# A gated linear attention whose decays come from a forward and a backward scan, feeding two MLPs: a change to how the decays are made and to the order of the opening

## The chip, the cores and the metric

The kernel runs on one core of a Trainium2 chip. The metric is the device time of one execution in microseconds (us). The engines are TensorE (PE in the profile, with PEld for its weight loads), VectorE (DVE), ScalarE (ACT), GpSimd (POOL) and SyncE (SP, which here only issues transfers). ACT issues transfers too; a transfer that an engine issues is marked with a q behind the engine's name (ACTq, SPq).

## The reference

```python
# q, k, v, f_logit: (4, 8, 768, 48), float32
f = 1 / (1 + exp(-f_logit))
for t in range(768):
    state = f[:, :, t, :, None] * state + k[:, :, t, :, None] * v[:, :, t, None, :]
    y[:, :, t] = einsum('bhd,bhde->bhe', q[:, :, t], state)
x = y as (3072 tokens, 384)
x = ((sigmoid(x @ w_gate)) * (x @ w_val)) @ w_out          # d_ff 1536
h = x @ w_in;  out = (h * sigmoid(1.702 * h)) @ w_out2     # d_ff 2048
```

## The kernel before, in words

The attention is cut into 48 units. A unit is one pair of heads (2 x 48 rows of state, laid on partitions 0 to 47 and 64 to 111) and 256 tokens, which are four chunks of C = 64 tokens. UG = 4 pairs make the 384 rows of x for 256 tokens, so units 0 to 3 make the first 256 tokens of x, units 4 to 7 the next.

For a unit, ACT takes the sigmoid of the gates (`forget`), DVE scans them into a running product that starts anew at each chunk (`begin_decay`, L804) and takes the reciprocal of all 256 products (`end_decay`, L811). POOL multiplies q by the products (`decay_q`, L506) and k by their reciprocals (`decay_k`, L514). `prepare(n)` on DVE is both steps, `decay(n)` on POOL both multiplications. `take_end` on ACT keeps each chunk's whole product in p_end; `prepare_q` multiplies q by the end of the chunk before.

TensorE does the attention in 50 visits. Visit v can do three things for three units (`VISITS[v]`): turn k of unit n and make its scores (it needs k_dec, then q_dec), make the chunks' key-value products of unit n-1, and make the outputs of unit n-2 (it needs the masked scores and the states, which DVE makes in `mask` and `new_states` after a visit, in `after_visit`). After some visits of the opening TensorE multiplies an identity on nothing (`keep_warm`: 8 times after visits 6 and 7). Visits 0 to 7 come ahead of the MLPs: visits 0 to 3 turn units 0 to 3, visit 4 makes the products of unit 3, visits 5 and 6 the outputs of units 2 and 3, and visit 7 turns unit 4.

Outputs y go by DMA into x_raw. The MLPs run behind it, block by block: a block is 128 hidden rows for one group of tokens (the first two groups have 256 tokens, the others 512). Every fp32 operand is split into a high part (ACT) and the rest (DVE, or POOL for the first weight piece and for w2), and each product is three matmuls (L1087 to L1089). TensorE's order in a block of the first MLP is: gate, value, a visit if one is due, and the output product of the block before. The sequences of all engines are written out by hand, one after another in each engine's function, so an instruction that waits holds back all that stands behind it on its engine. `PREPARE_AT`, `FORGET_AT` and `VISIT_AT` say in which blocks `prepare`, `forget` and the later visits stand. The gates' first two and the other loads of the opening stand in ACT's and SP's sequences.

The weights of the first MLP come in 12 pieces. Piece t is loaded by ACT (`load_w1`), cast (`w1_first_part`) and finished by DVE (`w1_second_part`), piece 0 in thirds by POOL (`split_w1`), and block 0 waits for these.

Of the kernel before, what the change touches and what calls it, by code (L numbers as in the profile page):

```python
# [12 lines left out]
P = 128  # L13
# [3 lines left out]
def gla_moe_moe2(nc, q_t, k_t, f_t, v_n, v_t, w1, w2, out_t, x_dram, x2_dram):  # L17
# [68 lines left out]
    with ExitStack() as ctx:  # L86
# [33 lines left out]
        gate = sb("gate", [P, 2, W])  # L120
        floor = sb("floor", [P, 2, W])
        prod = sb("prod", [P, 2, W])
        inv_prod = sb("inv_prod", [P, 2, W])
# [32 lines left out]
        gate_done = sem("gate_done")  # L156
        scan_done = sem("scan_done")
        inv_done = sem("inv_done")
# [148 lines left out]
        def end_before(u, c):  # L307

            return p_end[:, u.n, c - 1:c] if c else p_end[:, u.n - UG, CH - 1:CH]
# [57 lines left out]
        with nc.Block() as block:  # L367

            @block.sync
            def _(sp):  # L370
# [7 lines left out]
                def load_kq(n):  # L378
                    if n < UNITS:
                        u = Unit(n)  # L380
                        wait(sp, q_dec_done, n - 1)
                        for i in range(PAIR):
                            sp.dma_start(q_raw[rows[i], u.s, :], q_t[u.pair, i, :, u.tokens]).then_inc(q_loaded[u.s], 16)
                        wait(sp, k_dec_done, n - 1)
                        for i in range(PAIR):
                            sp.dma_start(k_raw[rows[i], u.s, :], k_t[u.pair, i, :, u.tokens]).then_inc(k_loaded[u.s], 16)
# [48 lines left out]
                move_y(3, slice(1, None))  # L435
                load_f(7)
# [49 lines left out]
            def _(pool):  # L486
# [8 lines left out]
                                   pattern=[[1, C]], channel_multiplier=-1).then_inc(steps_set, 1)  # L495
                pool.wait_ge(steps_set, 3)
# [3 lines left out]
                def decay_q(n):  # L500
# [5 lines left out]
                    pool.tensor_tensor(q_dec[:, n % 4, :], q_raw[:, u.s, :], prod[:, u.s, :], ALU.mult).then_inc(q_dec_done, 1)  # L506

                def decay_k(n):
                    u = Unit(n)
                    pool.wait_ge(k_loaded[u.s], (u.uses + 1) * 32)  # L510
                    pool.wait_ge(inv_done, n + 1)
                    if n >= 2:
                        pool.wait_ge(visit_done, turn_visit[n - 2] + 1)
                    pool.tensor_tensor(k_dec[:, u.s, :], k_raw[:, u.s, :], inv_prod[:, u.s, :], ALU.mult).then_inc(k_dec_done, 1)  # L514

                def decay(n):
                    if n < UNITS:
                        decay_q(n)
                        decay_k(n)
# [38 lines left out]
            def _(act):  # L558
# [19 lines left out]
                def forget(n):  # L578
# [7 lines left out]
                    f_c = f_raw[:, u.s, :].rearrange("p (c t) -> p c t", c=CH)  # L586

                    act.activation(gate[:, u.s, :].rearrange("p (c t) -> p c t", c=CH)[:, :, 1:C], f_c[:, :, 1:C], ACT.Sigmoid)
                    act.activation(floor[:, u.s, :].rearrange("p (c t) -> p c t", c=CH)[:, :, 0], f_c[:, :, 0],
                                   ACT.Sigmoid).then_inc(gate_done, 1)  # L590
# [18 lines left out]
                def take_end(n):  # L609

                    act.wait_ge(scan_done, n + 1)
                    act.copy(p_end[:, n, :],
                             prod[:, n % 2, :].rearrange("p (c t) -> p c t", c=CH)[:, :, C - 1]).then_inc(p_end_done, 1)

                def prepare_q(n):
# [44 lines left out]
                act.activation(y_t[:, 0, 0:1], x_raw[:, 0, 0:1], ACT.Sigmoid)  # L660
                first_load_f(1)
# [26 lines left out]
                first_load_f(6)  # L688
                load_w1(2)
# [4 lines left out]
                first_move_y(3, slice(0, 1))  # L694
                w1_first_part(1)
# [91 lines left out]
            def _(dve):  # L787

                dve.memset(f_raw[:, :, :], 30.0).then_inc(gaps_set, 1)
                dve.memset(q_raw[:, :, :], 0.0).then_inc(gaps_set, 1)  # L790
                dve.memset(k_raw[:, :, :], 0.0).then_inc(gaps_set, 1)
                dve.memset(gate[:, :, :], 0.0).then_inc(gaps_set, 1)
                dve.memset(floor[:, :, :], SAFE_PRODUCT).then_inc(gaps_set, 1)
                dve.memset(no_state[:, :], 0.0).then_inc(gaps_set, 1)
# [4 lines left out]
                def begin_decay(n):  # L799
                    u = Unit(n)  # L800
                    dve.wait_ge(gate_done, n + 1)
                    wait(dve, q_dec_done, n - 1)
                    wait(dve, p_end_done, n - 1)
                    dve.tensor_tensor_scan(prod[:, u.s, :], gate[:, u.s, :], floor[:, u.s, :], 1.0, ALU.mult,  # L804
                                           ALU.max).then_inc(scan_done, 1)

                def end_decay(n):
                    u = Unit(n)
                    dve.wait_ge(scan_done, n + 1)
                    wait(dve, k_dec_done, n - 1)  # L810
# [399 lines left out]
```

## Time and profile before

| | |
|---|---|
| median of 3 runs | 950.77 us (950.76 to 953.5) |
| the profiled execution | 953.08 us, of which the span of instructions is 951.0 us |
| TensorE busy | 934.9 us of the span |
| VectorE busy | 487.0 us |
| ScalarE busy | 375.3 us |
| GpSimd busy | 105.8 us |
| mean granted clock of TensorE | 0.996 |

Times below are microseconds from the start of the span unless marked otherwise. Busy time is time in which an engine has an instruction at work; the idle time in brackets stands before an instruction, with what ended it.

### The profile page before, as it was taken

How to read it: one execution, taken by the hardware profiler on the slowest of the kernel's cores; microseconds unless marked ns; L12 is line 12 of the kernel's file. 1: busy time of each engine (PE TensorE's matmuls, PEld its weight loads, DVE VectorE, ACT ScalarE, POOL GpSimd, SP SyncE). 2: the span in 40 equal slices, each digit the busy share in tenths (PEclk: the TensorE clock that was granted, in tenths of full speed). 3: DMA queues.
4: the chain of work that ended last, by engine and by line, in shares of the span. 5: the costliest groups of instructions: out<-in, count | busy, mean ns of one | idle time of the engine just before them, and what ended most of it. 6: DMA issues, size and time to landing. Idle time of an engine off the chain costs nothing.

```text
span 951.0 us, 18139 instructions
## 1 busy us (share of the span) xinstructions
PE 934.9 (98%) x7203; PEld 781.2 (82%) x7203; DVE 487.0 (51%) x829; ACT 375.3 (39%) x941; POOL 105.8 (11%) x125
## 2 busy tenths in 40 slices
PE   7899999999999999999999999999999999999997
PEld 5899988888888888888888888888888888888885
DVE  7897776647665665664333234343443443433433
ACT  4665444543444444443424333233232333232332
POOL 4211211101110111110004420000000000000000
PEclk9899999999999999999999999999999999999999
DMA  5762322211112212120123320020010200100000
GB/s 146 201 188 60 85 64 61 64 47 58 57 48 54 80 52 51 29 80 21 63 69 98 99 84 1 1 67 1 24 43 1 68 1 1 66 1 1 34 1 35
DMA packets 44008, 52.36 MB, mean 55 GB/s; under 512 B 8464, under 2 KB 33808, under 8 KB 43920
## 3 DMA queue, kind: packets, MB, share of 16 engines
q1 hardware_dynamic: 41184, 43.30, 15.8%
q10 hardware_dynamic: 2736, 7.85, 2.9%
q8 instruction: 59, 0.97, 0.4%
q14 instruction: 29, 0.24, 0.1%
HBM read 36.96 MB, written 9.44 MB: 49 GB/s over the span
## 4 chain that ended last, share of the span: by engine, by line
PE 95%; DVE 2%; issue 1%; ACT 1%; DMA 1%; SPq 0%; ACTq 0%; POOL 0%; DVEq 0%; POOLq 0%
PE up_ps L1087 17%; PE up_ps L1088 17%; PE up_ps L1089 17%; PE out_ps L1087 13%; PE out_ps L1088 12%; PE out_ps L1089 12%; PE att_ps L1035 2%; PE att_ps L1057 1%; PE att_ps L1047 1%; PE turn_ps L1014 1%; PE up_ps L1003 1%; PE att_ps L1069 1%; PE att_ps L1080 1%; DMA x_raw<-y_t 1%; DVE inv_prod L811 1%
## 5 line engine op out<-in xcount | busy, mean ns | idle before, releaser
L1087 PE MATMUL up_ps<-x_hi,w_hi 128*128 128x512 f32 (+1 forms) x792 | 293.7, 371 | 1.5 <-DVE x_lo L867 0.8
L1089 PE MATMUL up_ps<-x_hi,w_lo 128*128 128x512 f32 (+1 forms) x792 | 293.2, 370 | 0.0
L1088 PE MATMUL up_ps<-x_lo,w_hi 128*128 128x512 f32 (+1 forms) x792 | 293.1, 370 | 0.0
L1087 PE MATMUL out_ps<-act_hi,w_hi 128*128 128x512 f32 (+1 forms) x540 | 208.0, 385 | 0.8 <-DVE act_lo L932 0.8
L1088 PE MATMUL out_ps<-act_lo,w_hi 128*128 128x512 f32 (+1 forms) x540 | 203.2, 376 | 0.0
L1089 PE MATMUL out_ps<-act_hi,w_lo 128*128 128x512 f32 (+1 forms) x540 | 202.9, 376 | 0.0
L718 ACT CAST act_hi<-act_f 128x512 fp32r<-128x512 f32 (+1 forms) x180 | 106.6, 592 | 232.1 <-DVE act_f L923 159.7
L932 DVE TENSOR_TENSOR act_lo<-act_f,act_hi 128x512 fp32r<-128x512 f32 (+1 forms) x180 | 118.1, 656 | 113.8 <-ACT act_hi L718 113.8
L1087 PEld LDWEIGHTS up_ps<-x_hi,w_hi 128*128 128x128 f32 x792 | 149.7, 189 | 27.8 <-DVE x_lo L867 1.3
L1089 PEld LDWEIGHTS up_ps<-x_hi,w_lo 128*128 128x128 f32 x792 | 149.6, 189 | 25.3
L1088 PEld LDWEIGHTS up_ps<-x_lo,w_hi 128*128 128x128 f32 x792 | 149.7, 189 | 25.0
L926 DVE TENSOR_TENSOR act_f<-act_f,up_ps 128x512 f32<-128x512 f32 x96 | 66.0, 688 | 173.3 <-ACT act_f L714 173.3
L714 ACT ACTIVATE act_f<-up_ps 128x512 f32<-128x512 f32 x96 | 57.4, 598 | 192.9 <-PE up_ps L1089 192.9
L1087 PEld LDWEIGHTS out_ps<-act_hi,w_hi 128*128 128x128 f32 x540 | 101.8, 188 | 22.2 <-DVE act_lo L932 1.2
L1089 PEld LDWEIGHTS out_ps<-act_hi,w_lo 128*128 128x128 f32 x540 | 102.0, 189 | 18.6
L1088 PEld LDWEIGHTS out_ps<-act_lo,w_hi 128*128 128x128 f32 x540 | 102.0, 189 | 16.9
L923 DVE TENSOR_TENSOR act_f<-act_f,up_ps 128x512 f32<-128x512 f32 (+1 forms) x84 | 50.3, 599 | 112.5 <-PE up_ps L1089 103.9
L811 DVE RECIPROCAL inv_prod<-prod 128x256 f32<-128x256 f32 x48 | 84.1, 1752 | 1.6
L712 ACT ACTIVATE act_f<-up_ps 128x512 f32<-128x512 f32 (+1 forms) x84 | 45.1, 537 | 62.7 <-PE up_ps L1089 60.7
L506 POOL TENSOR_TENSOR q_dec<-q_raw,prod 128x256 f32<-128x256 f32 x48 | 35.3, 735 | 299.6 <-DVE prod L804 229.9
L639 ACT COPY y_t<-att_ps 48x128 f32<-48x128 f32 x128 | 33.3, 260 | 60.3 <-DVE state L840 59.2
L624 ACT ACTIVATE q_in<-q_dec,p_end 128x64 f32<-128x64 f32 x176 | 47.4, 339 | 0.9
(77 smaller groups left out, 577.7 us busy)
## 6 DMA issues: line engine op xcount, KB each, us to landing
stage<-w SPq DMA_DIRECT2D x16, 384.0 KB, 3.3
stage<-w ACTq DMA_DIRECT2D x9, 576.0 KB, 4.3
q_raw<-q_t SPq DMA_DIRECT2D x96, 48.0 KB, 1.9
k_raw<-k_t SPq DMA_DIRECT2D x96, 48.0 KB, 1.9
v_raw<-v_n SPq DMA_DIRECT2D x48, 96.0 KB, 2.2
x_raw<-x_dram SPq DMA_DIRECT2D x6, 768.0 KB, 5.0
out_t<-final SPq DMA_DIRECT2D x18, 256.0 KB, 2.1
f_raw<-f_t SPq DMA_DIRECT2D x82, 48.0 KB, 1.9
```

The costliest lines, as they stand in the source:

```text
L506: pool.tensor_tensor(q_dec[:, n % 4, :], q_raw[:, u.s, :], prod[:, u.s, :], ALU.mult).then_inc(q_dec_done, 1)
L624: last = act.mul(q_in[:, n % 2, at], q_dec[:, n % 4, at], end_before(u, c))
L712: act.activation(act_f[:, b.t, 0:b.n], up_ps[:, 0, 0:b.n], ACT.Sigmoid).then_inc(sig_done, 1)
L714: act.activation(act_f[:, b.t, 0:b.n], up_ps[:, b.j % 2, 0:b.n], ACT.Sigmoid, scale=1.702).then_inc(sig_done, 1)
L718: act.copy(act_hi[:, b.t, 0:b.n], act_f[:, b.t, 0:b.n]).then_inc(act_hi_done, 1)
L811: dve.reciprocal(inv_prod[:, u.s, :], prod[:, u.s, :]).then_inc(inv_done, 1)
L923: dve.tensor_tensor(act_f[:, b.t, 0:b.n], act_f[:, b.t, 0:b.n], up_ps[:, 1, 0:b.n], ALU.mult).then_inc(mul_done, 1)
L926: dve.tensor_tensor(act_f[:, b.t, 0:b.n], act_f[:, b.t, 0:b.n], up_ps[:, b.j % 2, 0:b.n], ALU.mult).then_inc(mul_done, 1)
L932: dve.tensor_tensor(act_lo[:, b.t, 0:b.n], act_f[:, b.t, 0:b.n], act_hi[:, b.t, 0:b.n].bitcast(F32), ALU.subtract).then_inc(act_split, 1)
L1087: pe.matmul(dst, w_hi[:, at:at + P], m_hi, start=first, stop=False)
L1088: pe.matmul(dst, w_hi[:, at:at + P], m_lo, start=False, stop=False)
L1089: return pe.matmul(dst, w_lo[:, at:at + P], m_hi, start=False, stop=last)
```

## The change

The product up to a token and its reciprocal are replaced by two scans. One runs backwards over the chunk and gives, for each token, the product of the gates behind it (`after_prod`), which k takes. The other runs forwards, but starts each chunk at one over the chunk's whole product, and q takes it (`to_prod`). Four reciprocals per unit, one for each chunk, are left of the 256. The buffers get two columns per chunk for the starts and ends (264 instead of 256 elements). The sigmoid is one instruction instead of two. On POOL, k comes before q. The states and q_in are decayed by the chunk's own product (`end_of`) instead of the one before. `begin_decay` is now the backward scan with the four reciprocals, `end_decay` the forward scan; in the MLP's blocks the first stands ahead of `after_visit`, the second behind it. The opening's sequences on SP, POOL, ACT and DVE are written anew.

```diff
@@ POOL
+pool.memset(starts[:, :, :], SAFE_PRODUCT).then_inc(starts_set, 1)
+pool.memset(no_state[:, :], 0.0).then_inc(starts_set, 1)
+pool.memset(starts[...][:, :, :, C + 1], 1.0).then_inc(starts_set, 1)
 def decay_q(n):
-    pool.tensor_tensor(q_dec[:, n % 4, :], q_raw[:, u.s, :], prod[:, u.s, :], ALU.mult)
+    pool.tensor_tensor(by_chunk(q_dec[:, n % 4, :]), by_chunk(q_raw[:, u.s, :]), chunks(to_prod, u.s)[:, :, 1:C + 1],
+                       ALU.mult)
 def decay_k(n):
-    pool.wait_ge(inv_done, n + 1)
-    pool.tensor_tensor(k_dec[:, u.s, :], k_raw[:, u.s, :], inv_prod[:, u.s, :], ALU.mult)
+    pool.wait_ge(after_done, n + 1)
+    pool.tensor_tensor(by_chunk(k_dec[:, u.s, :]), by_chunk(k_raw[:, u.s, :]), chunks(after_prod, u.s)[:, :, 2:],
+                       ALU.mult)
 def decay(n):
-        decay_q(n)
         decay_k(n)
+        decay_q(n)
 decay(3)
-pool.wait_ge(state_done, CH * 2)
 split_w1(0)
 split_w1(1)
+decay_k(4)
+split_w1(2)
 decay_q(4)
-pool.wait_ge(state_done, CH * 4)
-split_w1(2)
-decay_k(4)
 decay(5)
@@ ACT
-    act.activation(gate...[:, :, 1:C], f_c[:, :, 1:C], ACT.Sigmoid)
-    act.activation(floor...[:, :, 0], f_c[:, :, 0], ACT.Sigmoid).then_inc(gate_done, 1)
+    act.activation(chunks(gate, u.s)[:, :, 1:C + 1], by_chunk(f_raw[:, u.s, :]), ACT.Sigmoid).then_inc(gate_done, 1)
+act.wait_ge(gaps_set, 2)
 first_load_f(1)
 forget(0)
 first_load_f(2)
 forget(1)
-first_load_f(3)
 take_end(0)
 take_k(0)
+first_load_f(3)
 forget(2)
-first_load_f(4)
 take_end(1)
+take_k(1)
 prepare_q(0)
-take_k(1)
 forget(3)
 load_w1(0)
-prepare_q(1)
 take_end(2)
 take_k(2)
-first_load_f(5)
+prepare_q(1)
+take_end(3)
 w1_first_part(0)
+take_k(3)
 take_y(0)
-take_end(3)
-take_k(3)
+prepare_q(2)
 load_w1(1)
-prepare_q(2)
 forget(4)
 take_y(1)
 prepare_q(3)
-first_load_f(6)
-load_w1(2)
 forget(5)
 take_y(2)
 first_move_y(2, slice(2, None))
 take_y(3)
 first_move_y(3, slice(0, 1))
+load_w1(2)
 w1_first_part(1)
@@ SP: k before q in load_kq; load_f(4), load_f(5), load_f(6) added ahead of load_kq(4), load_kq(5) and load_f(7)
@@ DVE
-dve.memset(f_raw[:, :, :], 30.0)
+dve.memset(f_raw[:, 0, :], 30.0)
+dve.memset(f_raw[:, 1, :], 30.0)
-dve.memset(floor[:, :, :], SAFE_PRODUCT)
-dve.memset(no_state[:, :], 0.0)
 def begin_decay(n):
-    wait(dve, q_dec_done, n - 1)
-    dve.tensor_tensor_scan(prod[:, u.s, :], gate[:, u.s, :], floor[:, u.s, :], 1.0, ALU.mult, ALU.max)
+    wait(dve, k_dec_done, n - 1)
+    dve.tensor_tensor_scan(after_prod[:, u.s, ::-1], gate[:, u.s, ::-1], starts[:, u.s, ::-1], 1.0, ALU.mult, ALU.max)
+    dve.wait_ge(after_done, n + 1)
+    dve.reciprocal(chunks(starts, u.s)[:, :, 0], chunks(after_prod, u.s)[:, :, 1]).then_inc(start_done, 1)
 def end_decay(n):
-    wait(dve, k_dec_done, n - 1)
-    dve.reciprocal(inv_prod[:, u.s, :], prod[:, u.s, :]).then_inc(inv_done, 1)
+    wait(dve, q_dec_done, n - 1)
+    dve.tensor_tensor_scan(to_prod[:, u.s, :], gate[:, u.s, :], starts[:, u.s, :], 1.0, ALU.mult, ALU.max)
 prepare(0)
 prepare(1)
+begin_decay(2)
 after_visit(0)
-prepare(2)
+end_decay(2)
+begin_decay(3)
 after_visit(1)
-prepare(3)
+end_decay(3)
 after_visit(2)
-begin_decay(4)
 after_visit(3)
 after_visit(4)
-end_decay(4)
-begin_decay(5)
 w1_second_part(1)
+prepare(4)
 x_second_part(0)
+prepare(5)
 after_visit(7)
-end_decay(5)
@@ DVE, in a block of the first MLP
+    begin_decay(ahead)
     after_visit(v)
     take_out(b.group - 1)
-    prepare(PREPARE_AT[b.g, b.j])
+    end_decay(ahead)
```

## Rows read from the trace of the kernel before

**Rows 1.** The page: busy time, share of the span and instructions of each engine.
```profile
PE 934.9 (98%) x7203; PEld 781.2 (82%) x7203; DVE 487.0 (51%) x829; ACT 375.3 (39%) x941; POOL 105.8 (11%) x125
```

**Rows 2.** Busy time of each engine by stretch, then TensorE's granted clock and DMA.
```profile
24.30:27.70 3.40, 3.35 (x24) 3.21 (x25) 1.19 (x2) 1.85 (x5) 1.69 (x3) 0.50 0.81 226
...
41.30:44.70 3.40, 1.84 (x68) 1.42 (x66) 3.26 (x8) 1.83 (x5) 0.72 (x1) 1.00 0.76 222
44.70:48.10 3.40, 3.40 (x16) 3.40 (x17) 3.40 (x6) 2.44 (x11) 0.73 (x1) 0.51 0.16 18
...
50.00:100.00 50.00, 49.47 (x716) 47.26 (x716) 42.24 (x76) 27.00 (x81) 8.79 (x12) 1.00 0.41 116
...
230.00:460.00 230.00, 230.00 (x2306) 188.90 (x2305) 137.99 (x251) 103.58 (x324) 30.02 (x40) 1.00 0.19 53
```

**Rows 3.** The page: groups of instructions, busy time, mean ns, idle before.
```profile
L811 DVE RECIPROCAL inv_prod<-prod 128x256 f32<-128x256 f32 x48 | 84.1, 1752 | 1.6
L506 POOL TENSOR_TENSOR q_dec<-q_raw,prod 128x256 f32<-128x256 f32 x48 | 35.3, 735 | 299.6 <-DVE prod L804 229.9
```

**Rows 4.** TensorE in order of time, 0 to 60 us: start, duration, instruction, idle before.
```profile
1.39 8.30 PE L1003 MATMUL up_ps<-x_raw 128*128 128x384 f32 x16 [1.39 <-POOL x_raw L487]
9.52 0.38 PE L1014 MATMUL turn_ps<-ident,k_dec 128*128 128x128 f32 x2
...
22.97 0.44 PE L1035 MATMUL out_ps<-scores,v_raw 64*48 64x64 f32 x16 [2.38 <-DVE state L840]
...
25.16 3.25 PE L999 MATMUL up_ps<-ident 128*128 128x128 f32 x16
28.24 0.38 PE L1014 MATMUL turn_ps<-ident,k_dec 128*128 128x128 f32 x2
28.55 0.46 PE L1057 MATMUL att_ps<-q_dec,k_dec 48*64 48x64 f32 x16
28.94 2.05 PE L999 MATMUL up_ps<-ident 128*128 128x128 f32 x16
30.75 0.36 PE L1087 MATMUL up_ps<-x_hi,w_hi 128*128 128x256 f32 x1
...
32.39 0.39 PE L1087 MATMUL up_ps<-x_hi,w_hi 128*128 128x256 f32 x1 [0.60 <-DVE x_lo L867]
...
43.06 0.44 PE L1035 MATMUL att_ps<-scores,v_raw 64*48 64x64 f32 x16 [1.49 <-issue]
```

**Rows 5.** VectorE in order of time, 0 to 60 us.
```profile
20.21 0.69 DVE L804 TENSOR_TENSOR_SCAN prod<-gate,floor 128x256 f32<-128x256 f32 x1 [2.00 <-ACT floor L589]
20.82 0.40 DVE L822 TENSOR_TENSOR scores<-out_ps,causal 128x256 f32<-128x256 f32 x1
...
22.38 0.86 DVE L840 SCALAR_TENSOR_TENSOR state<-state,p_end,att_ps 128x48 f32<-128x48 f32 x3
...
28.13 1.36 DVE L874 TENSOR_TENSOR w_lo<-stage,w_hi 128x1152 fp32r<-128x1152 f32 x1 [2.64 <-ACT w_hi L569]
...
34.60 0.42 DVE L923 TENSOR_TENSOR act_f<-act_f,up_ps 128x256 f32<-128x256 f32 x1 [0.27 <-ACT act_f L712]
...
41.82 1.15 DVE L840 SCALAR_TENSOR_TENSOR state<-state,p_end,att_ps 128x48 f32<-128x48 f32 x4
```

**Rows 6.** ScalarE and its transfer issues in order of time, 0 to 60 us.
```profile
10.21 0.42 ACT L588 ACTIVATE gate<-f_raw 128x252 f32<-128x252 f32 x1
...
10.76 0.79 ACTq L602 DMA_DIRECT2D f_raw<-f_t  x2
...
23.70 0.45 ACTq L563 DMA_DIRECT2D stage<-w  x1
...
25.96 0.37 ACT L635 COPY y_t<-att_ps 128x256 f32<-128x256 f32 x1 [0.94 <-PE att_ps L1069]
...
26.95 1.15 ACT L569 CAST w_hi<-stage 128x1152 fp32r<-128x1152 f32 x1 [0.61 <-ACT y_t L635]
```

**Rows 7.** GpSimd in order of time, 0 to 60 us.
```profile
23.33 1.00 POOL L526 TENSOR_TENSOR w_lo<-stage,w_hi 128x384 fp32r<-128x384 f32 x1 [1.57 <-DVE state L840]
25.04 0.97 POOL L514 TENSOR_TENSOR k_dec<-k_raw,inv_prod 128x256 f32<-128x256 f32 x1 [0.71 <-issue]
```

More of the change, by code:

```diff
@@ L119, in gla_moe_moe2 @@
         v_raw = sb("v_raw", [P, 4, BLOCKS, E2])
[L120 to L123, printed above, removed]
+        SPACED = CH * (C + 2)
+        gate = sb("gate", [P, 2, SPACED])
+        after_prod = sb("after_prod", [P, 2, SPACED])
+        to_prod = sb("to_prod", [P, 2, SPACED])
+        starts = sb("starts", [P, 2, SPACED])
         q_dec = sb("q_dec", [P, 4, W])
@@ L305, in state_before, with chunks, by_chunk, end_of @@
             return state[:, (u.n - UG) % STATES, CH - 1, :] if u.third else no_state[:, :]
-        def end_before(u, c):
-            return p_end[:, u.n, c - 1:c] if c else p_end[:, u.n - UG, CH - 1:CH]
+        def chunks(spaced, s):
+            return spaced[:, s, :].rearrange("p (c t) -> p c t", c=CH)
+        def by_chunk(t):
+            return t.rearrange("p (c t) -> p c t", c=CH)
+        def end_of(u, c):
+            return p_end[:, u.n, c:c + 1]
         class Block:
@@ L380, in load_kq @@
                         u = Unit(n)
+                        wait(sp, k_dec_done, n - 1)
+                        for i in range(PAIR):
+                            sp.dma_start(k_raw[rows[i], u.s, :], k_t[u.pair, i, :, u.tokens]).then_inc(k_loaded[u.s], 16)
+                        if n == 0:
+                            sp.wait_ge(gaps_set, 4)
                         wait(sp, q_dec_done, n - 1)
@@ L429, in _ @@
                 load_v(3)
+                load_f(4)
                 load_kq(4)
+                load_f(5)
                 move_y(0)
@@ L495, in _ @@
                                    pattern=[[1, C]], channel_multiplier=-1).then_inc(steps_set, 1)
+                pool.memset(starts[:, :, :], SAFE_PRODUCT).then_inc(starts_set, 1)
+                pool.memset(no_state[:, :], 0.0).then_inc(starts_set, 1)
+                pool.wait_ge(starts_set, 2)
+                pool.memset(starts[:, :, :].rearrange("p s (c t) -> p s c t", c=CH)[:, :, :, C + 1], 1.0).then_inc(starts_set, 1)
                 pool.wait_ge(steps_set, 3)
@@ L609, in take_end @@
                 def take_end(n):
-                    act.wait_ge(scan_done, n + 1)
-                    act.copy(p_end[:, n, :],
-                             prod[:, n % 2, :].rearrange("p (c t) -> p c t", c=CH)[:, :, C - 1]).then_inc(p_end_done, 1)
+                    act.wait_ge(after_done, n + 1)
+                    act.copy(p_end[:, n, :], chunks(after_prod, n % 2)[:, :, 1]).then_inc(p_end_done, 1)
                 def prepare_q(n):
@@ L623, in prepare_q @@
                         at = slice(c * C, (c + 1) * C)
-                        last = act.mul(q_in[:, n % 2, at], q_dec[:, n % 4, at], end_before(u, c))
+                        last = act.mul(q_in[:, n % 2, at], q_dec[:, n % 4, at], end_of(u, c))
                     last.then_inc(q_in_done, 1)
@@ L839, in new_states @@
                         else:
-                            dve.scalar_tensor_tensor(out=after[:, c, :], in0=state_before(u, c), scalar=end_before(u, c),
+                            dve.scalar_tensor_tensor(out=after[:, c, :], in0=state_before(u, c), scalar=end_of(u, c),
                                                      in1=products, op0=ALU.mult, op1=ALU.add).then_inc(state_done, 1)
@@ L934, in _ @@
                     v = VISIT_AT.get((b.g, b.j)) if b.first_mlp else None
+                    ahead = PREPARE_AT.get((b.g, b.j), UNITS) if b.first_mlp else UNITS
+                    if ahead < UNITS:
+                        begin_decay(ahead)
                     if v is not None:
@@ L938, in _ @@
                         take_out(b.group - 1)
-                    if b.first_mlp and (b.g, b.j) in PREPARE_AT:
-                        prepare(PREPARE_AT[b.g, b.j])
+                    if ahead < UNITS:
+                        end_decay(ahead)
                     if b.first_mlp and b.g < NG1 - 1 and b.j == SPLIT_AT1:
```

36 lines of the change are left out of this document (17 added, 19 removed).

## The prediction

> **What bounds the kernel now.** I read the busy shares first. TensorE is busy 934.9 of 951.0 us, VectorE 487.0 [rows 1]. Then the stretches: from 230 to 460 us, in the middle of the attention, TensorE is busy in all 230.00 us, and from 50 to 100 us in 49.47 of 50.00 [rows 2]. VectorE has 42.24 us in that second stretch, a lot, and TensorE still hardly waits for it. So a cheaper VectorE is worth next to nothing after 50 us: less than the 0.53 us that TensorE is idle there. What can move is the start. The time lines show it: TensorE stands still before 22.97 (2.38 us), before 32.39 (0.60 us) and before 43.06 (1.49 us) [rows 4], and its clock is granted at half (1.2 instead of 2.4 GHz) from 24.3 to 27.7 and again from 44.7 to 48.1, each time after one of the longer pauses [rows 2]. Once the blocks of the MLP run without a gap, the end of the program is the start of the blocks plus a fixed amount of TensorE's work. So the question is when the first blocks run, compared with 30.75 us, and when visit 9 runs, compared with 43.06 us.
>
> **The change part by part.**
>
> *The decays.* The reciprocal of 256 columns takes 1.75 us [rows 3] and goes. Two scans stand where one stood. The scan takes 0.69 us for 256 columns [rows 5]; at 264 columns 0.69 x 264/256 = 0.71, with its gap 0.72. The new reciprocal of four columns has no row. From above it is the copy-like small operations: three state steps take 0.86 us [rows 5], so 0.29 each with 48 columns; from below it is 1.75 x 4/256 = 0.03 us. I take 0.14, the middle. A unit costs VectorE 0.72 + 0.14 + 0.72 = 1.58 us, before 0.72 + 1.67 (the reciprocal's 1.75 less the overlap with its neighbour) = 2.39. That saves 0.8 us per unit, 39 us over 48 units, nearly all of it under TensorE's work and worth nothing. That the reversed scan costs what the forward one does is an assumption; it could cost up to twice as much (0.7 us more), which is a rival below.
>
> *In a block of the first MLP* the backward scan and the four reciprocals (0.86 us) now stand ahead of `after_visit`, and so the masks and states come later by that. From 34.60 [rows 5] to visit 9 at 43.06 [rows 4] VectorE is never idle and TensorE waits for it. There one `prepare` (for unit 6) gets 0.8 us shorter, and 0.86 us is put ahead of the states of unit 4. These cancel: 8.46 us before, 8.5 us after. So the pause of 1.49 us before visit 9 is not shortened, and the half clock from 44.7 to 48.1 us probably comes again. In the later blocks the same 0.86 us delays masks and states, but visits there are at least 5 us apart by the order of the blocks, and TensorE was never idle from 230 to 460 us; I cost it at nothing. Were that cover gone, it would be at most 0.86 us for each of some 40 visits.
>
> *The very start.* TensorE multiplies to keep its clock up from 1.39 until visit 0 at 9.52 us [rows 4], and that is not changed. The shorter memsets and the earlier k (some 1 us) are hidden behind it. On ACT the load of unit 3's gates (two issues, 0.79 us for such a pair) now stands between the copy of the turned k and the sigmoid of unit 2, which stood at 10.21 [rows 6]; it goes to 10.85 and ends at 11.25.
>
> *Units 2 and 3.* From 11.25 on VectorE's sequence sets the pace: unit 2's decays and the mask of unit 0 (1.58 + 0.34) to 13.2; unit 3's backward scan with reciprocals, mask and states of the second visit and its forward scan (0.86 + 0.3 + 1.1 + 0.72) to 16.2; mask and states for unit 1 (1.45) to 17.6; TensorE ends visit 3 some 0.8 later, at 18.4; mask and states for unit 2 (1.45) to 19.85; states for unit 3 (1.05) to 20.9. Before, these last states ended at 22.38 + 0.86 = 23.24, since the scan of unit 4 stood ahead of them and itself waited 2.00 us for its gates [rows 5]. So this is 2.3 us earlier. The last y was copied at 25.96 [rows 6], 2.7 after the states; 20.9 + 2.7 = 23.6, perhaps 0.3 less because visit 6 runs at the full clock: 23.3. **Here the new order gains 2.6 us.**
>
> *From there to block 0.* The cast of weight piece 1 started 1.0 us after that copy (26.95); the weight load that was issued at 23.70 in 0.45 us now stands ahead of it [rows 6], so it starts at 23.3 + 1.0 + 0.45 = 24.75 and ends 1.15 later, at 25.9. On VectorE `prepare(4)` now stands behind `w1_second_part(1)`, which takes 1.36 us [rows 5] and needs this cast: 27.25. The backward scan of unit 4: 28.0. k of unit 4 on POOL takes 0.97 beside a scan [rows 7], not the 0.74 of its sister's mean [rows 3]: 28.95. Behind it stands the last third of piece 0, 1.00 us [rows 7]: 29.95. Then q, 0.75: 30.7. Visit 7 turns k at 28.95 and makes the scores at 30.7, to 31.1. Before, it had both at 28.24 and 28.55 [rows 4]. Then come the eight warm-up products, unchanged: 1.8 us at the full clock (28.94 to 30.75), 3.25 at half (25.16) [rows 4]. TensorE will have been idle since about 24.5, but for the two transposes: over 6 us, against pauses of 2.38 and 1.49 that brought half the clock. I take the half clock: block 0 starts at 34.4 us instead of 30.75; at the full clock it would be 32.9.
>
> *What block 0 gives back.* x is ready by then (the moves start earlier, at 23), so its stall of 0.60 us and the busy ACT behind it vanish: 18 matmuls of 0.12 us, 2.3 us to VectorE's product instead of the 3.85 from 30.75 to 34.60 [rows 4, 5]. That product comes at 36.7 instead of 34.6, or 35.2 at the full clock. Everything to visit 9 and to the end is carried along: **2.1 us later at the half clock, 0.6 at the full one.** I weigh the half clock at four fifths and take 1.9.
>
> *The contention.* k beside a scan took 0.97 us, against 0.74 otherwise [rows 3, 7]; both k and q now run beside scans more often. The Trainium skill, page GPSIMD Engine Reference, section Specifications, says that GpSimd shares its SBUF interfaces with VectorE, with contention when a VectorE instruction has two SBUF inputs. A scan has two and the reciprocal has one, so by that rule the change puts more of POOL's work under contention. By the row alone the sum has 0.23 us for k already; by the rule q would take the same more, 0.2 us.
>
> *Sum.* The profiled execution took 953.08 us around a span of 951.0; its span becomes 952.9, its time 955.0. The median of the runs is 2.3 us under the profiled time, so against it: 950.77 + 1.9 = **952.7 us**.
>
> **The rivals.**
> 1. *The clock stays up.* If TensorE runs the warm-up products at the full clock, 0.6 us are lost: 951.4. For it: the placing of the fall differs by microseconds. Against it: pauses of a quarter of this length brought it before.
> 2. *The gain of the opening reaches the blocks* (the other side of my forecast). If k and q of unit 4 are ready before TensorE asks, for instance because ACT's cast comes at 24 us and the third is no hindrance, block 0 starts at 31.0, its product comes at 33.3 instead of 34.6: 1.3 us gained; if also the pause before visit 9 stays without a half clock, 1.7 us more (3.4 us at half): 947.8. It decides where the scores of unit 4 can start by 28.9 us.
> 3. *Reversed scans are slow.* With 0.7 us more for each, one lies on the way to visit 7 and two (units 6 and 7) between 34.6 and 43.06: 2.1 us more, 954.8. Nothing in the trace shows a reversed scan.
> 4. *The relief of VectorE counts in the first groups after all*, in the 0.53 us idle from 50 to 100 us and the like after it: at most some 1 us, 951.7.
> 5. *A second half clock.* If the pause before visit 9 grows because TensorE arrives there sooner than VectorE, the half clock lasts longer: 1.7 us more, 954.4.
>
> **How the numbers follow.** Forecast, 952.7 us: 0.45, its own range 951.8 to 953.8. Rival 1: 0.17. Rival 4: 0.06. Rival 2: 0.13, of which 0.09 is faster by over 0.3%. Rivals 3 and 5: 0.10 and 0.09. A measurement of this kernel can tell about 0.3%, here 2.85 us: faster means under 947.9, slower over 953.6. Slower gets most of rivals 3 and 5 and a little of the forecast, 0.21; the same 0.70; faster 0.09. The range leaves out the full gain of rival 2 and the sum of rivals 3 and 5: 949.3 to 955.2.
>
> **What would show it.** Right: `starts`' reciprocal near 0.14 us and the backward scan near 0.71; the last states of the opening at 21 us; the last y at 23.3; `w_lo` of piece 1 before the scan of unit 4; visit 7's scores at 30.7, then L999 at 3.25 us and the first L1087 at 34.4; the pause before visit 9 about as long; 230.00 of 230.00 us busy in the middle. Wrong: the first L1087 under 32 us, a scan over 1 us, idle TensorE in the middle of the attention, or a clock at half in other places than these.

## The result, and the profile after

| | before | changed |
|---|---|---|
| median | 952.38 us (8 runs, 950.76 to 953.83) | 957.02 us (8 runs, 954.73 to 959.84) |
| the same, measured again | 952.12 us (30 runs) | 955.60 us (10 runs, 953.03 to 958.53) |
| profiled execution, span | 951.0 us | 954.0 us |
| mean granted clock of the profiled execution | 0.996 | 0.993 |

The ratio is 1.005, with a 95% interval of 1.0031 to 1.0068; measured again it is 1.0040 (1.0027 to 1.0053). The change is slower by 0.4 to 0.5%. The forecast was 952.7 us with a range of 949.3 to 955.2. Of the 4.3 us by which the median misses it, 1.6 us are the kernel before itself: its median is 952.4 over 8 runs, not the 950.77 of the first three. The other 2.7 us are the change's: 1.9 us were forecast for it and 4.6 measured.

First the page of the changed kernel: busy time by engine.

```profile
PE 935.8 (98%) x7203; PEld 783.1 (82%) x7203; DVE 455.9 (48%) x876; ACT 371.3 (39%) x893; POOL 102.7 (11%) x128
```

And the groups of the decays on VectorE: count, busy time and mean ns, idle before.

```profile
L827 DVE TENSOR_TENSOR_SCAN to_prod<-gate,starts 128x264 f32<-128x264 f32 x48 | 44.8, 932 | 0.9
L817 DVE TENSOR_TENSOR_SCAN after_prod<-gate,starts 128x264 f32<-128x264 f32 x48 | 33.6, 701 | 2.7 <-ACT gate L606 2.5
...
L820 DVE RECIPROCAL starts<-after_prod 128x4 f32<-128x4 f32 x48 | 8.7, 181 | 1.6
```

VectorE is relieved by 31 us, from 487.0 to 455.9 [rows 1], and the program is slower. TensorE has the same 7,203 matmuls, and is busy for 935.8 us instead of 934.9. So only the places where TensorE stands still or runs at the lower clock can tell. Where the two kernels differ in them is ahead of 60 us: from 60 to 150 us TensorE stands still for 0.95 us, before for 1.18, and from 150 to 900 us for nothing in either. TensorE in order of time, changed kernel:

```profile
1.39 6.98 PE L1023 MATMUL up_ps<-x_raw 128*128 128x384 f32 x16 [1.39 <-POOL x_raw L503]
...
21.30 2.05 PE L1019 MATMUL up_ps<-ident 128*128 128x128 f32 x16
27.38 0.44 PE L1034 MATMUL turn_ps<-ident,k_dec 128*128 128x128 f32 x2 [4.02 <-POOL k_dec L536]
29.46 0.70 PE L1077 MATMUL att_ps<-q_dec,k_dec 48*64 48x64 f32 x16 [1.64 <-POOL q_dec L526]
30.09 3.78 PE L1019 MATMUL up_ps<-ident 128*128 128x128 f32 x16
33.52 0.56 PE L1107 MATMUL up_ps<-x_hi,w_hi 128*128 128x256 f32 x1
...
42.96 0.38 PE L1034 MATMUL turn_ps<-ident,k_dec 128*128 128x128 f32 x2
45.53 0.68 PE L1055 MATMUL att_ps<-scores,v_raw 64*48 64x64 f32 x16 [2.19 <-issue]
```

Set against [rows 4]: visit 7 waits 4.02 us for k of unit 4 and 1.64 us more for its q, where it waited for neither before. The eight warm-up products behind it take 3.78 us instead of 2.05. Block 0 starts at 33.52 instead of 30.75, visit 9 at 45.53 instead of 43.06. What k of unit 4 was late for stands on VectorE:

```profile
19.06 0.86 DVE L856 SCALAR_TENSOR_TENSOR state<-state,p_end,att_ps 128x48 f32<-128x48 f32 x3
24.54 1.36 DVE L890 TENSOR_TENSOR w_lo<-stage,w_hi 128x1152 fp32r<-128x1152 f32 x1 [4.61 <-ACT w_hi L589]
25.81 0.70 DVE L817 TENSOR_TENSOR_SCAN after_prod<-gate,starts 128x264 f32<-128x264 f32 x1
...
26.76 1.12 DVE L827 TENSOR_TENSOR_SCAN to_prod<-gate,starts 128x264 f32<-128x264 f32 x1
...
36.81 0.42 DVE L940 TENSOR_TENSOR act_f<-act_f,up_ps 128x256 f32<-128x256 f32 x1 [3.69 <-PE up_ps L1109]
...
53.58 0.42 DVE L940 TENSOR_TENSOR act_f<-act_f,up_ps 128x256 f32<-128x256 f32 x1 [3.33 <-PE up_ps L1109]
```

The last states of the opening end at 19.9 us; before, at 23.24 [rows 5]. Then VectorE is idle for 4.61 us, in which it could have scanned unit 4, whose gates were there at 18.9 us:

```profile
18.52 0.41 ACT L606 ACTIVATE gate<-f_raw 128x256 f32<-128x256 f32 x1
```

It waits for the cast of weight piece 1, since `w1_second_part(1)` stands ahead of `prepare(4)`. On GpSimd the last third of piece 0 stands between unit 4's k and q:

```profile
26.65 0.68 POOL L536 TENSOR_TENSOR k_dec<-k_raw,after_prod 128x256 f32<-128x256 f32 x1 [7.26 <-issue]
27.28 1.39 POOL L549 TENSOR_TENSOR w_lo<-stage,w_hi 128x384 fp32r<-128x384 f32 x1
28.64 0.67 POOL L526 TENSOR_TENSOR q_dec<-q_raw,to_prod 128x256 f32<-128x256 f32 x1
```

The stretches, with the granted clock in the third column from the end, answer to [rows 2]:

```profile
27.70:31.10 3.40, 1.76 (x22) 1.56 (x21) 1.64 (x5) 2.26 (x5) 1.61 (x2) 0.61 0.81 204
31.10:34.50 3.40, 3.40 (x17) 3.40 (x17) 1.95 (x4) 1.54 (x6) 1.36 (x2) 0.50 0.86 274
...
44.70:48.10 3.40, 2.49 (x64) 2.25 (x64) 3.33 (x7) 0.84 (x4) 0.68 (x1) 0.62 0.32 115
48.10:51.50 3.40, 3.40 (x19) 3.34 (x16) 1.71 (x6) 2.68 (x7) 0.00 (x0) 0.50 0.57 138
...
230.00:460.00 230.00, 230.00 (x2365) 189.01 (x2365) 124.54 (x272) 101.42 (x304) 28.14 (x40) 1.00 0.20 53
```

So the clock is at 1.2 GHz in two places: over the warm-up products and the start of block 0, and behind the pause of 2.19 us, now for longer. In the kernel before the first lower stretch lay ahead of visit 7, and block 0 then had to wait 0.60 us for x [rows 4], so it can have cost little there. From 230 to 460 us TensorE is busy in all 230.00, as before.

The balance of the two profiled executions: VectorE's product of block 0 is 2.21 us later (34.60 to 36.81), visit 9 2.47 us later, the product of block 3 3.86 us later (49.72 to 53.58). The span is 3.0 us longer; VectorE's last copies to the output start 3.46 us later (944.63 to 948.09), so 0.4 us of the 3.9 come back before the end and 0.5 us in the last few microseconds; neither was followed up.

### The profile page after: what moved, and what is told of

The parts are those of the page before. It is cut to its first block, busy times and chain, and to the rows that moved or that the text cites. A ratio compares the mean times of both kernels' runs of the same rounds, so it can differ in the third digit from the quotient of the medians.

```text
span 954.0 us, 18139 instructions
## 1 busy us (share of the span) xinstructions
PE 935.8 (98%) x7203; PEld 783.1 (82%) x7203; DVE 455.9 (48%) x876; ACT 371.3 (39%) x893; POOL 102.7 (11%) x128
## 3 DMA queue, kind: packets, MB, share of 16 engines
HBM read 36.96 MB, written 9.44 MB: 49 GB/s over the span
## 4 chain that ended last, share of the span: by engine, by line
PE 95%; DVE 1%; DMA 1%; SPq 1%; issue 1%; ACT 0%; POOL 0%; ACTq 0%; DVEq 0%; POOLq 0%
PE up_ps L1107 17%; PE up_ps L1108 17%; PE up_ps L1109 17%; PE out_ps L1107 13%; PE out_ps L1108 12%; PE out_ps L1109 12%; PE att_ps L1055 2%; PE att_ps L1077 1%; PE att_ps L1067 1%; PE turn_ps L1034 1%; PE att_ps L1089 1%; PE att_ps L1100 1%; PE up_ps L1023 1%; DMA stage<-w 0%; SPq L414 0%
## 5 line engine op out<-in xcount | busy, mean ns | idle before, releaser
L536 POOL TENSOR_TENSOR k_dec<-k_raw,after_prod 128x256 f32<-128x256 f32 x48 | 33.3, 694 | 283.2 <-DVE after_prod L817 238.5
L654 ACT COPY y_t<-att_ps 48x128 f32<-48x128 f32 x128 | 33.3, 260 | 72.5 <-DVE state L856 71.4
L856 DVE SCALAR_TENSOR_TENSOR state<-state,p_end,att_ps 128x48 f32<-128x48 f32 x170 | 44.7, 263 | 4.9
```

Of the source, the lines that this page charges most:

```text
L536: pool.tensor_tensor(by_chunk(k_dec[:, u.s, :]), by_chunk(k_raw[:, u.s, :]), chunks(after_prod, u.s)[:, :, 2:], ALU.mult).then_inc(k_dec_d ...
L856: dve.scalar_tensor_tensor(out=after[:, c, :], in0=state_before(u, c), scalar=end_of(u, c), in1=products, op0=ALU.mult, op1=ALU.add).then_ ...
```

## The experiments

All ran beside the kernel before. Each line's ratio is to it; the interval is 95%. e1 to e4 ran on another chip than the other experiments; the kernel before took 952.18 us there, and 951.95 and 952.12 us beside the others.

| run | what | median us | ratio | interval |
|---|---|---|---|---|
| | changed kernel, first | 957.02 | 1.0050 | 1.0031 to 1.0068 |
| e11 | changed kernel, again | 955.60 | 1.0040 | 1.0027 to 1.0053 |
| e1 | opening orders of before | 950.62 | 0.9994 | 0.9979 to 1.0009 |
| e2 | unit 4 first | 951.26 | 1.0002 | 0.9991 to 1.0012 |
| e3 | no products behind visit 7 | 953.82 | 1.0019 | 1.0010 to 1.0028 |
| e4 | 26 products behind visit 6 | 954.15 | 1.0020 | 1.0008 to 1.0033 |
| e5 | states first | 954.62 | 1.0021 | 1.0012 to 1.0030 |
| e10 | products inside visit 9 | 954.87 | 1.0024 | 1.0014 to 1.0034 |
| e6 | e2 and e5 | 950.18 | 0.9974 | 0.9964 to 0.9983 |
| e9 | e2, e3 and e5 | 950.66 | 0.9983 | 0.9974 to 0.9992 |
| e7 | e1 and e5 | 948.67 | 0.9965 | 0.9952 to 0.9977 |
| e12 | e7 again | 949.75 | 0.9976 | 0.9966 to 0.9987 |
| e8 | e7, q before k in the blocks | 949.29 | 0.9971 | 0.9962 to 0.9981 |

### Is it the arithmetic or the order of the opening? (e1)

```diff
 # SP, POOL, ACT and DVE, up to the first block: the sequences of the kernel before, but
-decay_q(4)
+decay_k(4)
 pool.wait_ge(state_done, CH * 4)
 split_w1(2)
-decay_k(4)
+decay_q(4)
```

These lines are shown against the kernel before: unit 4's k and q keep the new arithmetic's order, k first. The shorter memsets and SP's loads of k before q also stay as in the changed kernel.

> The new arithmetic (two scans, four reciprocals, k before q, the scan ahead of the states in a block) with the opening orders of the kernel before on all four engines. Chain theory (the loss comes from the new opening order, which puts unit 4 behind the cast of weight piece 1 and runs the warm-up products at half clock): first L1107 near 30.8 us as in the kernel before, the first gate-value product on VectorE near 34.6, visit 9 at 43.1 to 44, time within 1.5 us of the kernel before. Arithmetic theory (the slower scans beside GpSimd and the work put ahead of the states lose the time): at least 3 us slower than before, with visit 9 past 45.

Measured: 950.62 us, ratio 0.9994. With the old opening the loss is gone, so it is the opening's and not the arithmetic's. TensorE in e1:

```profile
28.32 0.38 PE L1037 MATMUL turn_ps<-ident,k_dec 128*128 128x128 f32 x2
...
41.78 0.44 PE L1058 MATMUL att_ps<-scores,v_raw 64*48 64x64 f32 x16 [1.92 <-issue]
```

Visit 7 is at 28.32 without a wait, as it was at 28.24 [rows 4], and visit 9 even comes at 41.78, 1.3 us before the 43.06 of the kernel before, since block 0's product was ready 1.3 us earlier (33.34, not 34.60). The arithmetic theory, which wanted visit 9 past 45 and at least 3 us, is out. The median hides a spread: seven of e1's 12 executions took 948.1 to 950.7 us with a mean clock of 0.994 or 0.995, five took 953.5 to 955.1 with 0.990 or 0.991. The traced one (949.3 us) is of the first kind.

### Which part of the opening? (e2)

```diff
 # DVE
-w1_second_part(1)
 prepare(4)
+w1_second_part(1)
 # POOL
 decay_k(4)
-split_w1(2)
 decay_q(4)
+split_w1(2)
```

> The changed kernel with prepare(4) ahead of w1_second_part(1) on VectorE, and q of unit 4 ahead of the last third of weight piece 0 on GpSimd. Chain theory: visit 7 near 23.5 to 24 us instead of 27.4 and 29.5, block 0 bound by the last x_lo near 30.5 to 31, the first gate-value product near 34 instead of 36.8, about 2.5 to 3 us faster than the changed kernel and no slower than before by more than 1.5 us. Arithmetic theory and states theory: block 0 earlier, but visit 9 not earlier than 45 and the time unchanged from the changed kernel (957).

Measured: 951.26 us, ratio 1.0002. Two pairs of lines change places and the whole loss is gone. TensorE in e2:

```profile
27.59 0.38 PE L1034 MATMUL turn_ps<-ident,k_dec 128*128 128x128 f32 x2
...
42.31 0.44 PE L1055 MATMUL att_ps<-scores,v_raw 64*48 64x64 f32 x16 [2.00 <-issue]
```

Visit 7 no longer waits for k or q; it starts when the products behind visit 6 end (27.59, and not at 23.5 as expected, since in this execution the opening ran at half clock: 0.50 from 17.5 to 24.3 us). Block 0's product comes at 33.39. The chain theory holds. Both exchanges were made at once, so how much each is worth is not shown.

### How much of it is the clock? (e3, e4)

```diff
-keep_warm({0: 2, 1: 5, 2: 2, 4: 2, 6: 8, 7: 8}.get(v, 0))
+keep_warm({0: 2, 1: 5, 2: 2, 4: 2, 6: 8}.get(v, 0))          # e3
+keep_warm({0: 2, 1: 5, 2: 2, 4: 2, 6: 26, 7: 8}.get(v, 0))   # e4
```

> The changed kernel without the eight warm-up products behind visit 7 (nothing of the output depends on them). Chain theory: block 0 starts 3.4 us earlier, near 30.2 to 30.9, but its first matmuls run at half clock (0.21 us each instead of 0.12), so the first gate-value product comes near 34.3 to 34.8 instead of 36.8: 2 to 2.5 us faster than the changed kernel. Rival (the half clock alone is what costs, and the warm-up products are what ends it): the half clock lasts longer into the blocks, and the time is not better than the changed kernel's 957.

Measured: 953.82 us, ratio 1.0019. That is 1.8 us under the changed kernel's second median and 3.2 under its first; the chain theory gave 2 to 2.5. In its profiled execution, the fastest of its 12 (951.89 us), the clock was at 0.50 from 31.1 to 34.5 us, and still block 0's product came at 34.58 instead of 36.81. At this place, where the products didn't bring the clock up before block 0, they were only a delay.

> The changed kernel with 26 instead of 8 warm-up products behind visit 6, so that TensorE is busy until visit 7's transposes near 27.3 us. If the pause of 4 us before visit 7 is what brings the half clock: the eight products behind visit 7 take 1.8 us instead of 3.8, block 0 starts near 31.9, the first gate-value product near 34.3 to 34.6: 2.2 to 2.5 us faster than the changed kernel. If the clock falls for the second pause (1.6 us before the scores of unit 4) anyway: no gain.

Measured: 954.15 us, ratio 1.0020. The time is near what the first theory said, but the mechanism is not. The pause before visit 7 was filled, and yet the products behind visit 7 took 3.32 us. Block 0's product came at 37.89 us, 1.1 us later than in the changed kernel, where 34.3 to 34.6 was expected. TensorE ahead of these products:

```profile
29.29 0.44 PE L1034 MATMUL turn_ps<-ident,k_dec 128*128 128x128 f32 x2 [0.25 <-POOL k_dec L536]
31.58 0.46 PE L1077 MATMUL att_ps<-q_dec,k_dec 48*64 48x64 f32 x16 [1.85 <-POOL q_dec L526]
```

The clock fell behind the second pause, of 1.85 us, in which TensorE waited for q (0.71 from 31.1 to 34.5 us, 0.79 to 37.9). This opening was also slower by itself (cast of piece 1 at 25.26, changed kernel 23.35), and behind visit 9 the clock stayed up. All nine executions averaged a clock of 0.992 or more, with a median of 0.994; the changed kernel's 18 have a median of 0.990. So the gain goes with a higher clock over the executions, but the one that was traced doesn't show where it comes from. What it shows is that filling the first pause alone didn't keep the clock up over the products.

### The scan ahead of the states (e5, e6, e7, e12)

```diff
-if ahead < UNITS:
-    begin_decay(ahead)
 if v is not None:
     after_visit(v)
+if ahead < UNITS:
+    begin_decay(ahead)
```

> The changed kernel with one move in the blocks: begin_decay(ahead) behind after_visit(v) instead of ahead of it. Theory: from the first gate-value product (36.8 us in the changed kernel) to visit 9 (45.5) VectorE sets the pace, and 0.8 to 0.9 us of scan and reciprocals lie ahead of the states of unit 4. Moved behind them, visit 9 starts 0.85 us earlier and the pause before it falls from 2.2 to 1.35 us; the half clock behind it may get shorter. Time 0.9 to 2.5 us under the changed kernel, still slower than before. Rival (the pause is hidden or filled by another wait): no change in the time and the same pause.

Measured: 954.62 us, ratio 1.0021, 1.0 us under the changed kernel's second median (955.60). The pause before visit 9 is 1.38 us instead of 2.19, 0.81 less, as expected, and the clock is not lowered behind it in the profiled execution (but neither is it in e11's, behind 2.19 us):

```profile
47.70 0.44 PE L1055 MATMUL att_ps<-scores,v_raw 64*48 64x64 f32 x16 [1.38 <-issue]
```

That execution has block 0's product at 39.79, with TensorE at half clock from about 17 to 27 us and again over the products; visit 9 follows it by 7.91 us, against 8.72 in the changed kernel.

> The new arithmetic, the opening orders of the kernel before, and the states ahead of the backward scan in the blocks (e1 with the move of e5). Theory: visit 9 another 0.85 us earlier than in e1; 949.5 to 950, at or a little under the kernel before. Rival (VectorE's relief is worth nothing once TensorE is busy): equal to e1 within 0.3 us.

> The kernel of e7 once more, for its interval: 948.5 to 949.5 us, 0.25 to 0.4% under the kernel before. If e7's five times were a lucky choice: within 0.1% of the kernel before.

Measured: 948.67 and 949.75 us, ratios 0.9965 and 0.9976: faster than both kernels, twice, with intervals clear of 1. From block 0's product to visit 9 it is 7.91 us in both traces, and 8.46 in the kernel before [rows 4, 5]: there VectorE's relief counts. Against e1 the medians are 0.9 to 2.0 us lower. But the shorter seven of e1 have a median of 949.3 us, no higher than these, and none of e7's and e12's 13 executions is over 951. So what the move took away is mostly e1's longer executions (953.5 us and more). That the shorter pause before visit 9 (1.39 us, e1 1.92) does it is likely and not shown: none of e1's longer ones was traced.

> The changed kernel with unit 4's decays ahead of weight piece 1 and of the last third (as e2) and the states first (as e5). If the two add up, as the chain theory has it: about 1 us under e2, near 950.3 and 0.1 to 0.2% under the kernel before. If VectorE's relief before visit 9 is hidden once block 0 starts early: equal to e2, 951.3.

Measured: 950.18 us, ratio 0.9974. The new opening too beats the kernel before once unit 4 comes first and the states aren't held up. The two repairs add up: 0.4 to 0.5% for e2, 0.28% for the states (e5 against the changed kernel: 0.2 to 0.3%). In the traced execution unit 4 is early, and now block 0 waits for x, 4.1 us in two waits, the clock falls there, and its product comes at 34.86, no earlier than the 34.60 of the kernel before:

```profile
29.06 0.36 PE L1107 MATMUL up_ps<-x_hi,w_hi 128*128 128x256 f32 x1 [2.58 <-DVE x_lo L883]
...
31.17 0.58 PE L1107 MATMUL up_ps<-x_hi,w_hi 128*128 128x256 f32 x1 [1.52 <-DVE x_lo L883]
```

Its gain lies behind it: from there to block 3's product it is 13.80 us, before 15.12.

### All three together (e9)

```diff
 # e2 and e5, and
-keep_warm({... 6: 8, 7: 8}.get(v, 0))
+keep_warm({... 6: 8}.get(v, 0))
```

> The new opening order mended in three places: unit 4's decays ahead of weight piece 1 and of the last third (as e2), states first (as e5), no warm-up products behind visit 7 (as e3). If the losses add up: e2 is at 951.3, states first gives 0.85 more and the missing products nothing or little, since block 0 waits for x: 949.5 to 951. If the half clock comes for the longer pause ahead of block 0: 952 or more.

Measured: 950.66 us, ratio 0.9983. Taking the products away too gains nothing over e6 (0.9974; the intervals overlap): block 0 waits for x in both (2.3 us in two waits for x_lo here, 4.1 in e6), so the products stand in a time that is free.

### The pause before visit 9 alone (e10)

```diff
 last.then_inc(k_turned, 1)
+if v == 9:
+    for _ in range(8):
+        pe.matmul(out_ps[:, 2, 384:512], ident[:, :], ident[:, :], start=False, stop=False,
+                  skip_group_check=True)
```

> The changed kernel with eight products on the identity inside visit 9, behind its transposes, into a part of PSUM that nothing reads. They fill 1.8 of the 2.2 us in which TensorE waits for the states. If the pause is what brings the second half clock (0.62 of the clock from 44.7 to 48.1 us and 0.50 to 51.5 in the changed kernel), it is gone or shorter: VectorE's product of block 3, at 53.6 us, comes 1.4 to 3 us earlier, visit 9 itself does not move against the product of block 0, and the time falls by 1.5 to 2.5 us against the changed kernel. Rival (the clock falls for another reason, or the pause does not matter): the same time.

Measured: 954.87 us, ratio 1.0024, against 1.0040 for the changed kernel beside it (e11, 955.60 us). The intervals overlap a little, so the medians alone don't settle it. The single executions say a little more: seven of the changed kernel's 18 took over 957 us (three of the ten beside e10), none of e10's 11 took over 956.3, and its clock never averaged under 0.990. Its time line shows the pause filled and the clock up, but e11's, with the pause open, has the clock up too: block 3's product follows block 0's by 13.90 us here and by 13.89 there. So that the open pause is what brings the half clock is made likely by the spread, and not shown. TensorE in e10:

```profile
45.09 1.95 PE L1038 MATMUL out_ps<-ident 128*128 128x128 f32 x16
47.44 0.44 PE L1059 MATMUL att_ps<-scores,v_raw 64*48 64x64 f32 x16 [0.41 <-issue]
```

> The changed kernel itself once more, beside the experiments on the same chip: 955 to 958 us, 0.4 to 0.6% over the kernel before, with a lower mean granted clock in the slower executions.

Measured: 955.60 us, and seven of the ten executions averaged a clock of 0.990 or less. The profiled one shows how uneven the changed kernel is. It has the same pause of 2.19 us before visit 9 and no lower clock behind it. It lost its time earlier, in an opening at half clock:

```profile
17.50:20.90 3.40, 3.13 (x52) 2.55 (x48) 1.71 (x7) 2.37 (x9) 1.95 (x2) 0.50 0.63 188
20.90:24.30 3.40, 2.90 (x57) 2.36 (x57) 0.53 (x2) 1.47 (x6) 0.00 (x0) 0.50 0.33 89
```

Block 0's product is at 39.37 there, 2.56 us after that of the first profile, and block 3's 13.89 us later:

```profile
39.37 0.42 DVE L940 TENSOR_TENSOR act_f<-act_f,up_ps 128x256 f32<-128x256 f32 x1 [4.19 <-PE up_ps L1109]
...
53.26 0.42 DVE L940 TENSOR_TENSOR act_f<-act_f,up_ps 128x256 f32<-128x256 f32 x1 [0.88 <-PE up_ps L1109]
```

In the first profile it is 16.77 us later. The difference, 2.88 us, is the price of the half clock behind visit 9 where it comes in full. In the traces in which it comes for a shorter time the distance is 15.12 us (the kernel before), 15.37 (e3) and 15.59 (e2), and in all the others 13.6 to 13.9. The pauses before visit 9 don't sort them: 1.49, 1.89 and 2.00 us with a lower clock behind, 1.92 (e1) and 2.19 (e4, e11) without one. The two traced executions of the changed kernel lose the same, 955.72 and 955.41 us, in two ways: one behind visit 9, the other in the opening. An execution with both would take some 958.3 us by these numbers (955.72 + 2.56, an estimate); seven of the 18 took 958.0 to 959.8, but none of them was traced.

### Who slows the forward scan? (e8)

```diff
 # POOL, in the blocks
-decay(PREPARE_AT[g, j])
+decay_q(PREPARE_AT[g, j])
+decay_k(PREPARE_AT[g, j])
```

> As e7, and in the blocks GpSimd multiplies q before k, so that k's product does not run beside the forward scan. Contention theory: the forward scan falls from 1.12 to 0.70 us in the blocks, since GpSimd is idle beside it, and visit 9 comes up to 0.4 us earlier; q's and k's products then run beside the next instruction of VectorE, and w_lo stays at 1.8. Rival (the forward scan is slow for itself, because it goes through the starts): it stays at 1.1.

Measured: 949.29 us, ratio 0.9971, no different from e7. The contention theory holds for the scan, and the time goes elsewhere: visit 9 follows block 0's product by 7.97 us, in e7 by 7.91. The group of the forward scan in e8 (busy time and mean ns, idle before):

```profile
L831 DVE TENSOR_TENSOR_SCAN to_prod<-gate,starts 128x264 f32<-128x264 f32 x48 | 35.3, 735 | 1.4
```

VectorE in order of time, in e8:

```profile
37.05 1.81 DVE L894 TENSOR_TENSOR w_lo<-final,w_hi 128x1152 fp32r<-128x1152 f32 x1
38.79 0.91 DVE L953 TENSOR_TENSOR act_lo<-act_f,act_hi 128x256 fp32r<-128x256 f32 x1
```

And GpSimd, in e8:

```profile
36.96 0.69 POOL L523 TENSOR_TENSOR q_dec<-q_raw,to_prod 128x256 f32<-128x256 f32 x1 [4.75 <-DMA q_raw<-q_t]
37.61 1.80 POOL L533 TENSOR_TENSOR k_dec<-k_raw,after_prod 128x256 f32<-128x256 f32 x1
```

The forward scan falls from a mean of 1,062 ns (e7) to 735. But k's product, 0.68 us in the changed kernel, takes 1.80 beside w_lo, and act_lo takes 0.91 instead of 0.41.

Read the starts: it is each time the instruction that starts second that gets longer. q starts at 36.96 and keeps 0.69, w_lo starts 0.09 us later and takes 1.81 instead of 1.35; k starts beside w_lo and takes 1.80; act_lo starts beside k and takes 0.91. The changed kernel has it too. There k of unit 4 starts at 26.65 and the forward scan at 26.76, and it is the scan that pays. For an earlier unit the backward scan starts first, at 11.98, and q's product pays (0.93 instead of 0.68 us); VectorE, then GpSimd:

```profile
11.98 0.68 DVE L817 TENSOR_TENSOR_SCAN after_prod<-gate,starts 128x264 f32<-128x264 f32 x1
```

```profile
12.20 0.93 POOL L526 TENSOR_TENSOR q_dec<-q_raw,to_prod 128x256 f32<-128x256 f32 x1 [0.71 <-DVE to_prod L827]
```

So exchanging k and q moved the cost to others and took nothing of it away.

## Why the prediction was wrong

The chain up to block 0 was right in its order and its waits. The profile has the last states at 19.9 (forecast 20.9), the last y at 21.67 (23.3), the cast at 23.35 (24.75), w_lo at 24.54 and behind it the backward scan at 25.81 (27.25), k, third and q in this order, the scores of visit 7 at 29.46 (30.7), the products at half clock (3.78 us, forecast 3.25) and block 0 at 33.52 (34.4). Everything ahead of block 0 is 0.9 to 1.6 us early; visit 0, which follows the first warm-up products, already was: 8.21 us instead of 9.52 [rows 4]. That block 0's product then came at 36.81, where 36.7 was forecast, is luck. The forecast gave block 0 2.3 us at the full clock, and it took 3.29, since the half clock lasted into its first matmuls (0.89 from 34.5 to 37.9 us); two errors of a microsecond cancel. e2 and e1 show that without this chain nothing is lost: with unit 4 first, or the old opening, the ratio is 1.0002 and 0.9994.

The forecast for the change was 1.9 us, and 4.6 and 3.5 us were measured. Three sizes were off, in one direction.

*The step "everything to visit 9 and to the end is carried along: 2.1 us later".* It held to visit 9 (2.47 us). It failed behind it. I took the pause before visit 9 to stay at 1.49 us, because the changes on VectorE between block 0's product and the states cancel. They nearly do: 8.46 us became 8.72. But TensorE arrives sooner. Its stall ahead of block 1 in the kernel before was gone, so it needed 6.15 us from block 0's product to the transposes of visit 9 (36.81 to 42.96) and not 6.6. Both together make 2.19 us. So TensorE's earlier arrival gave 0.45 us of the longer pause, and VectorE 0.26: there `prepare` got only 0.37 us shorter and not 0.8, because the forward scan takes 1.14 us beside k. The prediction had just this as rival 5, "if TensorE arrives there sooner than VectorE", with a chance of 0.09 and 1.7 us. In the profile the product of block 3 was then 3.86 us late, where 2.1 us were to be carried along: 2.21 at block 0, and 1.65 for the longer half clock. Where that comes in full its price is 2.9 us (the first profile against e11). That the longer pause is what made the half clock longer is not shown; e11 has the same pause and none.

*The clock of the opening.* "Here the new order gains 2.6 us" was reckoned at the full clock. In the profiled executions of e5, e10 and e11 the stretch from 17.5 to 24.3 us is at 0.50, w_lo of piece 1 starts at 27.2 to 28.1 instead of 24.5, and block 0's product is 1.9 to 3.0 us later than in the first profile. e2 and e9 have the same half clock in that stretch and block 0's product at 33.39 and 33.12, so it is unit 4's place behind this cast that has made the start of the blocks depend on it. The medians differ by more (3.5 and 4.6 us) than the first profiled spans (3.0 us); executions in which this delay and the one behind visit 9 come together would explain it, but none of over 957 us was traced.

*The basis.* The median of three, 950.77, lay 1.6 us under the median of eight. The mean granted clock of single executions of the kernel before ranges from 0.991 to 0.998, with times from 950.5 to 953.8; so a forecast made on three runs has this uncertainty on both sides of its range.

The rest, point by point. The backward scan is no dearer than the forward one (701 ns at 264 columns; forecast 710), so rival 3 is out. The four reciprocals take 0.18 us (0.14; the middle of the bounds 0.03 and 0.29 would have been 0.16). The forward scan takes 1.12 to 1.15 us beside k's product and 0.70 alone; the prediction had the contention on GpSimd's side, 0.23 us on k, and it is VectorE's scan that pays 0.42 us while k takes 0.68. The rule of the Trainium skill (GPSIMD Engine Reference, Specifications), that the two contend when VectorE's instruction has two SBUF inputs, agrees with this trace: beside the scans and w_lo, which have two, VectorE's instruction or GpSimd's gets longer, and the mask of scores, which takes one operand from PSUM, where TensorE's results are, keeps 0.39 us beside k's product (43.97). By the starts, it is the later of the two that pays (e8). Between block 0 and visit 9 it costs 0.4 us on the forward scan, of which 0.2 come back in w_lo. The last third took 1.39 us beside the forward scan, not 1.00. VectorE's relief was forecast at 39 us and is 31, since the forward scan has a mean of 932 ns and not 720. Rival 1 (the clock stays up over the products) didn't happen. Rival 2 named the right condition, k and q of unit 4 ahead of TensorE: e6, which meets it and has the states first, is at 950.18 us, 0.26% under the kernel before, less than the 0.3% or more that most of its chance went to; in its trace block 0 then waits for x, and its product comes at 34.86 and not at 33.3. Rival 4 is not seen in the changed kernel. From block 0's product to visit 9 it is 8.72 us there, before 8.46, and 7.91 with the states ahead of the scan (e5, e7): the relief counts there only if the scan isn't ahead of the states.

What stays open: why the opening runs at the full clock in one execution and at half in another, with the same instructions; why the clock falls behind visit 9 in some executions only; what goes on in the longest executions of the changed kernel and of e1, none of which was traced; and why e4 gained its 0.2 to 0.3%.

## What to carry to other kernels

When an order written by hand is rewritten, look at what each engine does in its idle time before its next wait. Here VectorE stood idle for 4.6 us with unit 4's gates ready, because an instruction that waited for a late cast stood in front, and exchanging two lines there and two on GpSimd gave back 0.4 to 0.5% of the whole program.

A relief of an engine off the critical path is worth what its first late product gains. With the old opening, 31 us less work gave nothing (0.9994) until the states were put ahead of the new scan (0.9976 and 0.9965), a move of one block of code.

A pause can cost twice: once for its length, and again at half clock behind it. Here pauses of 1.5 to 2.2 us before visit 9 had a half clock behind them in some executions and none in others, and it cost up to 2.9 us where it came. So give such a pause both outcomes in a forecast, and take the kernel's own spread from more than three runs.

## What the runs showed of the hardware

- A scan with a negative step on all three operands runs at the speed of the forward one: 701 ns for 128x264, where 128x256 forward took 682.
- When a VectorE instruction with two operands in SBUF overlaps one of GpSimd, the one that starts second gets longer, in every such pair shown here. A forward scan of 264 columns takes 0.70 us alone and 1.12 us when it starts 0.11 us behind GpSimd's product of 128x256, which keeps its 0.68 us. The product takes 0.93 us when it starts 0.22 us behind a scan, and 1.80 us when it starts 0.56 us behind a subtraction of 128x1152 (e8).
- GpSimd's product of 128x256 with one operand in chunks of 64 out of rows of 66 takes 0.68 us alone, no more than the plain one (0.72 to 0.74).
- TensorE's clock fell to 1.2 GHz behind a pause of 1.85 us (e4) and one of 1.49 us (the kernel before), and did not fall behind one of 2.19 us in another execution (e11).
